# Dummy matmuls left out of the early attention of an attention, gated MLP and expert kernel

## The reference

```python
# attention: q, k, v are (4, 8, 576, 64)
scores = scale * np.matmul(q, k.transpose(0, 1, 3, 2))
# heads 0-3: the last 32 positions; heads 4-7: earlier positions with the same residue mod 32
scores = np.where(masks[None, :, :, :], scores, -1000000000.0)
scores = scores - np.max(scores, axis=-1, keepdims=True)
attn = np.exp(scores)
attn = attn / (np.sum(attn, axis=-1, keepdims=True) + 1e-09)
x = np.matmul(attn, v)                       # -> (2304, 512)
# gated MLP, d_ff 1536
xn = x / rms * rms_g
g = xn @ w_gate
x = (g * sigmoid(g) * (xn @ w_val)) @ w_out
# 8 experts (512 -> 1024 -> 512), one per token
logits = x @ w_gate + modality_bias[modality_id]
e_idx = np.argmax(logits, axis=1)
out[mask] = gate_w[mask, None] * (np.maximum(x[mask] @ w1[e], 0.0) @ w2[e])
```

## Time and profile before

| | |
|---|---|
| time, median of 3 runs | 872.52 us (872.29 to 872.88) |
| span of the profiled execution | 870.5 us, 15612 instructions |
| what lies around the span, against the median | 2.0 us |
| TensorE busy | 857.1 us (98%), 5233 matmuls |
| VectorE busy | 520.7 us (60%) |
| ScalarE busy | 374.4 us (43%) |
| GpSimd busy | 328.4 us (38%) |
| DMA | 103.40 MB, mean 119 GB/s |
| mean granted TensorE clock | 0.997 of full speed |

### The profile page before, as it was taken

The page is one execution under the profiler, slowest core; times in us unless marked ns, Lnnn a source line. Parts: engine busy times, 40 slices in busy tenths (PEclk is TensorE's granted clock), DMA queues, the critical chain, the costliest instruction groups (busy, mean ns, idle before and its releaser), DMA issues.

```text
span 870.5 us, 15612 instructions
## 1 busy us (share of the span) xinstructions
PE 857.1 (98%) x5233; PEld 736.4 (85%) x5242; DVE 520.7 (60%) x1401; ACT 374.4 (43%) x945; POOL 328.4 (38%) x372
## 2 busy tenths in 40 slices
PE   8999999999999999999999999999999999999997
PEld 5678898888888888899999999988888888888885
DVE  6985555333453335449778763883877457666663
ACT  6966313545464455443321132243356235554442
POOL 3736762344323443356335333170043221222211
PEclk9999999999999999999999999999999999999999
DMA  9983212212223210242121121526265645555531
GB/s 191 289 212 88 61 48 65 84 55 78 53 60 112 52 38 27 71 157 74 42 93 61 61 73 37 210 81 254 97 205 206 241 144 191 184 213 182 192 128 39
DMA packets 77517, 103.40 MB, mean 119 GB/s; under 512 B 38973, under 2 KB 43069, under 8 KB 77312
## 3 DMA queue, kind: packets, MB, share of 16 engines
q1 hardware_dynamic: 73760, 91.16, 33.9%
q0 software_dynamic: 3680, 11.28, 3.7%
HBM read 92.98 MB, written 10.22 MB: 119 GB/s over the span
## 4 chain that ended last, share of the span: by engine, by line
PE 89%; DVE 8%; issue 1%; ACT 1%; POOL 1%; DMA 1%; SPq 0%; DVEq 0%; POOLq 0%; ACTq 0%
PE ps L1243 32%; PE ps L1282 16%; PE ps L1805 13%; PE ps L1790 13%; PE ps L1174 3%; PE ps L1203 2%; PE ps L1815 2%; PE ps L1184 2%; PE ps L1150 2%; PE ps L660 1%; DVE sm L1520 1%; DVE w_lo L2041 1%; DMA qk<-in_k 1%; PE ps L1312 1%; DVE h_lo L1600 1%
## 5 line engine op out<-in xcount | busy, mean ns | idle before, releaser
L1035 POOL TENSOR_TENSOR sm<-sm,rinv 72x288 f32<-72x288 f32 (+1 forms) x51 | 45.5, 893 | 174.2 <-DVE rinv L1531 174.1
L1067 POOL TENSOR_TENSOR out_lo<-out_raw,out_hi 128x512 fp32r<-128x512 f32 x72 | 101.8, 1414 | 5.8
L1589 DVE SCALAR_TENSOR_TENSOR h<-h,ps 128x384 f32<-128x384 f32 x72 | 39.8, 553 | 104.2 <-ACT h L1437 103.3
L1243 PE MATMUL ps<-x_hi,val_hi 128*128 128x384 f32 x288 | 101.1, 351 | 0.0
L1243 PE MATMUL ps<-x_hi,gate_hi 128*128 128x384 f32 x288 | 100.5, 349 | 0.4 <-DVE h L1589 0.4
L1065 POOL CAST out_hi<-out_raw 128x512 fp32r<-128x512 f32 x72 | 50.0, 694 | 135.0 <-DMA out_raw<-in_moe_w_out 135.0
L1441 ACT ACTIVATE h_hi<-h 128x384 fp32r<-128x384 f32 x72 | 37.8, 525 | 138.7 <-DVE h L1595 138.7
L1243 PE MATMUL ps<-x_hi,gate_lo 128*128 128x384 f32 x288 | 97.1, 337 | 0.0
L1243 PE MATMUL ps<-x_hi,val_lo 128*128 128x384 f32 x288 | 96.6, 336 | 0.0
L1243 PE MATMUL ps<-x_lo,val_hi 128*128 128x384 f32 x288 | 96.5, 335 | 0.0
L1243 PE MATMUL ps<-x_lo,gate_hi 128*128 128x384 f32 x288 | 93.9, 336 | 0.0
(11 more groups left out here) (278 smaller groups left out, 1947.5 us busy)
## 6 DMA issues: line engine op xcount, KB each, us to landing
w_raw<-in_moe_w SPq DMA_DIRECT2D x72, 512.0 KB, 4.9
out_raw<-in_moe_w_out SPq DMA_DIRECT2D x72, 256.0 KB, 2.6
x_rows<-y_tiles SPq DMA_DIRECT2D x18, 256.0 KB, 2.7
early_w_raw<-in_moe_w SPq DMA_DIRECT2D x8, 512.0 KB, 7.6
gate_raw<-in_moe_w_gate SPq DMA_DIRECT2D x4, 768.0 KB, 9.1
val_raw<-in_moe_w_val SPq DMA_DIRECT2D x4, 768.0 KB, 10.5
qk<-in_q SPq DMA_DIRECT2D x8, 288.0 KB
qk<-in_k SPq DMA_DIRECT2D x8, 288.0 KB
```

The source lines that it names most:

```text
L1035: pool.tensor_tensor(s3, s3, rinv[0:n, i, :].unsqueeze(2).to_broadcast([n, 4, c]), ALU.mult).then_inc(s_no, 1)
L1067: pool.tensor_tensor(ol[i][:, :], o_raw[i][:, :], oh[i][:, :].bitcast(f32), ALU.subtract).then_inc(s_ol, 1)
L1243: mm = pe.matmul(ps[:, bank, 0:CH], w[:, i, kk, cols], x[:, kk, :], start=(m == 0), stop=(m == n - 1))
L1589: dve.scalar_tensor_tensor(out=hf[n % 2][:, :], in0=hf[n % 2][:, :], scalar=1.0, in1=ps[:, 0, 0:CH], op0=ALU.add, op1=ALU.mult).then_inc(s ...
```

## The change

The dummies at a tick's end are issued only in ticks 0, 1 and 16 to 19 (SS[0] is 16). In ticks 2 to 15 the two matmuls are gone. Those before tick 0 and inside it stay.

```diff
                 if s >= EARLY:
                     for key in QK_AT.get(s, []):
                         turn_qk(*key)
-                if s < EARLY:
+                if s < 2 or SS[0] <= s < EARLY:
                     keep_busy({16: 3, 17: 3, EARLY - 1: 4}.get(s, 2))
```

## The result

The changed kernel takes 883.04 us (median of 4 runs, 881.42 to 886.50), the kernel before beside it 872.4 us (872.05 to 872.88): ratio 1.0123 with a 95% interval of 1.0105 to 1.0141, so 10.6 us slower where 2.0 us faster was forecast. Of each kernel's runs the ratios leave out those over 1.5% above its fastest, so a ratio can lie nearer to 1 than the two medians do. The profiled run took 882.35 us, its span is 880.6 us (870.5 before).

The account below looks back on a forecast made before the run. No single engine bounds the early attention; waits name TensorE for most of ticks 3 to 14, ScalarE close behind. ScalarE's waits, 1.11 plus 0.9, give 2.0 us: 872.5 - 2.0 = 870.5 us, 8 in 10 range 868.8 to 873.8.

Parts of the forecast that it names:

- The clock: Part on TensorE's granted clock without dummies in the early ticks: expected 1.00 up to 50 us, the only possible loss.
- the stretch that held: Earlier trace, 42.74 to 46.15 us: values, three dummies, scores, narrow matmuls, hardly a transpose; the clock stays at 1.00.
- the one that fell: Earlier trace from 602.4 us: 24 matmuls of 8 moving columns, then 8 transposes; clock 0.50 from 606 to 609 us.
- The weakest place: For the clock, ticks 14 and 15: they last 2.2 to 2.9 us whatever TensorE does, and it has time to spare.
- Rival 1: Clock falls again and again in ticks 4 to 13; half of the ten ticks hit, about 877.5 us; chance 0.14.
- ScalarE's waits, 2.0 us: The gain: ScalarE's waits for TensorE in the early ticks, 1.11 us before L1398 plus 0.9 us of shorter gaps.
- This stretch moves as a whole: From 36.7 us VectorE and GpSimd are both full; the stretch moves with what starts it, so ticks 14 and 15 add nothing.
- The stall: VectorE's 96x4 addition at 38.09 us, 0.81 us, ending with GpSimd's copy; claimed to become neither longer nor shorter.
- The rule on transposes: Trainium skill: transposes don't count for TensorE's clock as matmuls do; weighed against the change, over a third of a bare tick.
- Ticks 14 and 15 count nothing: From 36.7 us no gain is counted for these ticks, since VectorE and GpSimd are both full there.
- the q/k of batch 1: Nearest load behind the early stage: k lands about 52.3 us, is turned at 54.29; 2.0 us of slack, just enough.
- its issue moves forward as well: The batch 1 q/k load is issued earlier too where it hangs on q/k transposes, helping keep the slack.

Follow-up runs that it names:

- e6: Changed kernel with four float32 matmuls of 8 moving columns in the dummies' place in each of ticks 2 to 15; 903.76 us, ratio 1.0367.
- e3: Changed kernel with four 128x128 transposes in the dummies' place in each of ticks 2 to 15; 872.87 us, ratio 1.0011.
- e2: Kernel before with the dummies left out of ticks 2 to 7 and 12 to 15 only; 874.14 us, ratio 1.0015.
- e7: Changed kernel with one dummy put back in each of ticks 2 to 15; 872.66 us, ratio 1.0006.
- e8: The changed kernel run again, unaltered; 882.33 us over 10 runs (873.09 to 886.23), ratio 1.0085.
- e9: Changed kernel with VectorE's low parts of the first gate block moved from ticks 9 and 10 to 11 and 12; 880.12 us, ratio 1.0112.
- e13: Kernel before without dummies in ticks 8 to 11, VectorE's low parts of the first gate block moved to ticks 11 and 12; 873.51 us, ratio 1.0015.
- e5: Kernel before with the dummies left out of ticks 4 to 7, 11 and 12 only; 871.53 us, ratio 0.9989.
- e11: Second set of times of the kernel before with dummies left out of ticks 4 to 7, 11 and 12 only; 870.95 us, ratio 0.9993.
- e15: Kernel before without dummies in ticks 4 to 7, 11 and 12, with three in tick 3, four in 10, five in 15; 871.06 us, ratio 0.9985.
- e1: Kernel before with the dummies left out of ticks 2 to 7 only; 875.35 us, ratio 1.0016.
- e12: Kernel before with the dummies left out of ticks 8 to 11 only; 876.00 us, ratio 1.0048.

## Why the prediction was wrong

- **The step that failed** is in "The clock": "That is more like the stretch that held than like the one that fell." I compared what kinds of instruction a bare tick has with the two stretches of the earlier trace rows and passed over that the stretch that held, 42.74 to 46.15, has three dummies in it, the very instructions that the change takes out. A bare tick 10 or 11 has neither dummies nor q/k transposes: from the scores at 23.77 to those at 25.59, and again to those at 28.14, there are four score, four transposed-probability and four value products. Such ticks did not hold the clock: it fell to 0.50 behind them at 28 us and stayed there to 65 us, and the gate product came 11.66 us later. e6 shows a fall with records completely busy, e3 the clock held when four 128x128 transposes a tick are put back. Which of the waits and the missing work tips it in a single execution stays open.
- **The weakest place was named, but not the dearest.** The prediction saw it in ticks 14 and 15. In five profiled runs (e2, e7, e8, e9, e13) the clock did go at 41 to 43 us, behind a wait of 1.1 to 1.9 us in front of tick 16's scores, in e13 with the dummies of ticks 12 to 15 in place. But a short fall there costs little: e2's median is 1.4 us above that of the kernel before (874.14 against 872.74). The expensive ticks are 8 to 11, where the order in front of the prediction already showed a tick without q/k transposes, and where VectorE is 97% busy (9.38 of 9.70 us in the earlier trace rows), so that TensorE, done sooner, must wait for it: 0.20, 0.35, 1.08 us. The gain of the first ticks turned into a wait at the worst place. The prediction named what VectorE delays but did not ask what TensorE's own idle time does to its clock.
- **Rival 1 had the mechanism, not the size.** It priced five hit ticks at 1.2 us, 877.5 us. Its price per tick was near (a local tick 3.94 us against 2.63, 1.31 more; forecast 1.55). But in the profiled run one fall lasts 37 us: nothing behind it brought the clock back before the gate products, so ticks 12 to 19 paid as well, and the gate product came 11.7 us later. In e8, where the fall came at 41 us and lasted 10, 1.2 us won at tick 16 had become 2.7 us lost at the gate product: about 4 us.
- **ScalarE's waits, 2.0 us: right in sum, in part by luck.** In the run whose clock held to 41 us (e8), 1.9 us were won up to tick 14, and ScalarE's round was 1.81 us, as forecast. But 1.2 us of it lay ahead of tick 11's scores, where 0.5 to 1 us was forecast, and 0.7 behind them, where 1.5 was.
- **"This stretch moves as a whole": mis-sized.** The stall was put at 0.8 us and measured 1.30 in e8, so 1.2 us of the 2.0 came through to tick 16, the 1.2 that tick 9 had already set. It is GpSimd's copy that ends it (36.38 + 1.47 = 37.85, the addition 36.56 + 1.30 = 37.86), and that did not move forward as much as VectorE did. The Trainium skill's rule ("SBUF — State Buffer", section "Who interferes with whom"), by which the holder of the shared port pair blocks the other for a whole instruction, agrees with these ends; what I drew from it, that the stall keeps its length, does not follow: it grows by as much as VectorE comes too early. A gain of about 1.2 us at a held clock, an estimate from e8, is what the gate products of e5, e11 and e15 show (1.05 to 1.25 us), though these drop fewer dummies.
- **The rule on transposes does not explain it.** The prediction weighed the Trainium skill's rule ("TensorE: Matmul & The Clock Gate", section "Part 4: PE-mode transpose") that transposes don't count for the clock in the way matmuls do. e3 does not agree: with 4 transposes instead of the 2 dummies its profiled clock is 1.00 through the whole early attention, and the time is 872.87 us, not 883.
- **"Ticks 14 and 15 count nothing" held, the q/k of batch 1 only mostly.** In e8 the wait in front of tick 16 grew to 1.66 us, so these ticks gave nothing further. The load of q and k cost the changed kernel nothing, but "its issue moves forward as well" does not always hold: in e5's profiled run it moved 3.3 us back, and TensorE waited 0.82 us.

What stays open: what makes one execution of the same program hold (e8's at 873.9 us, half of e1's) and another fall. The timelines of e1 and of the changed kernel agree to 0.01 us in their waits around 15 us, and those of e8 and the changed kernel in theirs up to 28 us; one fell, the other did not. Nor was it tried to give TensorE useful work in place of the dummies in ticks 9 and 10.

## What to carry to other kernels

A matmul without a reader can be worth more than its 0.27 us: before leaving it out, look for the place where the engine behind it is full, since the time won there becomes TensorE's idle time. Do not take a full busy column, or a likeness in the kinds of instruction, as a sign that the clock will hold: look for a stretch without the dummies that did. Price a fall of the clock by the time until it comes back in a trace (4 to 37 us here, 57 in e6), not by the ticks that caused it. And take the median of many runs: three runs of e1 could have had a median of 870.4 or of 886.3 us.

## What the hardware showed unexpectedly

- TensorE at 100% busy in the records can lose its clock: with four narrow float32 matmuls (8 moving columns) added to each tick it fell at 17.9 us and stayed down until 75 us (0.50 still in 74 to 75), 903.76 us in all.
- Transposes of 128x128 float32 held it (e3, 1.00 from 9 to 60 us).
- Once at 1.2 GHz, a TensorE without a gap in its records (7.96 of 7.96 us busy) stayed there for 37 us; sixteen 128x512 bf16 matmuls in a row brought it back within their 5.2 us. One pair of dummies a tick took longer: 18 us in e1 (from 27.5 to 46.0), 10 us in e12 (from 35.1 to 44.8).
- Kernels whose early clock had fallen did not always fall again at 606 us: the changed kernel kept 1.00 there, where the kernel before had 0.50, and in e8 it was 0.76. In e11 and e15 both places held. That an early fall spares the later one is not shown.
